# Two tile gates moved to VectorE, and the other gates' matmuls moved between two transposes

## The reference

```
scores = scale * q @ k^T, masked to a window (4 heads) or a dilated window (4 heads)
x      = softmax(scores) @ v                      # 2304 rows of 512
logits = normed(x) @ normed(expert_emb)^T / tau   # 8 experts
e, g   = argmax(logits), softmax(logits)[argmax]
x      = g * (relu(x @ w1[e]) @ w2[e])            # per row, its one expert
h      = x @ w_in
out    = (h * cos(h)) @ w_out
```

## Time and profile before

| | |
|---|---|
| time, median of 3 executions | 856.87 us (856.0 to 858.98) |
| time of the profiled execution | 854.68 us |
| its span, first to last instruction | 852.8 us |
| TensorE busy | 823.2 us, 97% of the span |
| VectorE busy | 608.7 us, 71% |
| ScalarE busy | 489.9 us, 57% |
| GpSimd busy | 75.7 us, 9% |
| mean granted TensorE clock | 0.994 of full speed |

### The profile page before, as it was taken

The page is one execution under the profiler, slowest core; times in us unless marked ns, Lnnn a source line. Parts: engine busy times, 40 slices in busy tenths (PEclk is TensorE's granted clock), DMA queues, the critical chain, the costliest instruction groups (busy, mean ns, idle before and its releaser), DMA issues.

```text
span 852.8 us, 15550 instructions
## 1 busy us (share of the span) xinstructions
PE 823.2 (97%) x5046; PEld 753.6 (88%) x5046; DVE 608.7 (71%) x1187; ACT 489.9 (57%) x948; POOL 75.7 (9%) x129
## 2 busy tenths in 40 slices
PE   7999999989999999999999999999999999999994
PEld 5778787879999999999989999989999998999993
DVE  7888887876555555555577777798777788777762
ACT  4567767644455454444466666676666676666652
POOL 3112112240100000000000000011000003000002
PEclk9999999999999999999999999999999999999998
DMA  7597886255535434434431211223121214122001
GB/s 148 121 223 180 192 192 197 64 151 170 185 124 162 148 123 125 148 128 144 124 100 52 73 63 62 73 89 111 51 75 50 75 49 149 55 70 67 9 1 74
DMA packets 114913, 93.79 MB, mean 110 GB/s; under 512 B 65816, under 2 KB 94488, under 8 KB 114848
## 3 DMA queue, kind: packets, MB, share of 16 engines
q1 hardware_dynamic: 109920, 78.81, 32.5%
q0 software_dynamic: 4928, 14.16, 5.0%
HBM read 83.51 MB, written 9.44 MB: 109 GB/s over the span
## 4 chain that ended last, share of the span: by engine, by line
PE 84%; DVE 6%; issue 3%; DMA 2%; ACT 2%; POOL 1%; another core or an unknown queue 0%; POOLq 0%; DVEq 0%; ACTq 0%; SPq 0%
PE bank L765 24%; PE bank L763 24%; PE bank L764 24%; PE bank L625 2%; PE bank L604 2%; DMA xtok<-x_rows 2%; PE bank L613 1%; PE bank L588 1%; DVE shifted L1271 1%; DVE row_max L1268 1%; PE bank L706 1%; ACT probs L947 1%; PE bank L805 1%; DMA x_rows<-osb 1%; DVE kT L334 1%
## 5 line engine op out<-in xcount | busy, mean ns | idle before, releaser
L763 PE MATMUL bank<-yh,up_l 128*128 128x384 f32 x384 | 129.4, 337 | 0.5 <-DVE yl L1619 0.5
L765 PE MATMUL bank<-yh,up_h 128*128 128x384 f32 x384 | 129.5, 337 | 0.0
L764 PE MATMUL bank<-yl,up_h 128*128 128x384 f32 x384 | 128.9, 336 | 0.0
L765 PE MATMUL bank<-dn_h,hid 128*128 128x512 f32 x288 | 113.9, 396 | 0.0
L763 PE MATMUL bank<-dn_h,hid 128*128 128x512 f32 x288 | 112.5, 391 | 1.4 <-DVE hid L1597 1.4
L764 PE MATMUL bank<-dn_l,hid 128*128 128x512 f32 x288 | 113.8, 395 | 0.0
L1344 DVE TENSOR_TENSOR dn_l<-dn_raw,dn_h 128x512 fp32r<-128x512 f32 (+1 forms) x79 | 71.8, 909 | 54.5 <-ACT dn_h L998 52.5
L1141 ACT ACTIVATE work<-bank 128x384 f32<-128x384 f32 x96 | 47.2, 492 | 79.7 <-PE bank L765 78.7
L998 ACT ACTIVATE dn_h<-dn_raw 128x512 fp32r<-128x512 f32 (+1 forms) x79 | 63.7, 806 | 41.8 <-PE bank L765 41.8
L1153 ACT ACTIVATE work<-work 128x384 f32<-128x384 f32 x96 | 50.5, 526 | 63.8 <-DVE work L1592 61.8
L763 PE MATMUL bank<-xh,up_l 128*128 128x352 f32 x256 | 83.9, 328 | 2.0 <-DVE XS L1479 1.0
(11 more groups left out here) (212 smaller groups left out, 1692.4 us busy)
## 6 DMA issues: line engine op xcount, KB each, us to landing
up_raw<-in_moe_w_dram SPq DMA_DIRECT2D x32, 512.0 KB, 3.6
dn_raw<-in_moe_w_dram SPq DMA_DIRECT2D x32, 512.0 KB, 3.6
up_raw<-in_moe_w_in_dram SPq DMA_DIRECT2D x24, 512.0 KB, 3.4
dn_raw<-in_moe_w_out_dram SPq DMA_DIRECT2D x24, 512.0 KB, 3.6
qn<-in_q_dram SPq DMA_DIRECT2D x32, 144.0 KB, 2.9
kn<-in_k_dram SPq DMA_DIRECT2D x32, 144.0 KB, 3.3
xtok<-x_rows SPq DMA_DIRECT2D x4, 1152.0 KB, 7.6
x_rows<-osb POOLq DMA_DIRECT2D x8, 288.0 KB, 3.5
```

The lines of the kernel that those rows point to most:

```text
L763: mm(o, w[1], x[0], start=first, stop=False, skip_group_check=True)
L764: mm(o, w[0], x[1], start=False, stop=False, skip_group_check=True)
L765: return mm(o, w[0], x[0], start=False, stop=last, skip_group_check=True)
```

## The change

- The gates of tiles 0 and 2 are multiplied in by VectorE, with a `tensor_scalar`, in place of ScalarE. A semaphore `tile_gated_d` tells TensorE of them. Tile 1 and tiles 3 to 17 stay with ScalarE.
- On VectorE `to_gates(to_gate, rest)` goes ahead of `gates_out(head)`, and `ids_out(rest)` stands between the two new gate instructions. The four table instructions come after all of these.
- On TensorE the 24 matmuls with `to_gate` stand between the transposes of tiles 1 and 2, in place of after tile 2. One of the two `fill(1)` is gone.
- On VectorE `expert_up_lo(0, 1)` stands ahead of the wait for, and the read of, the rest's gates.

```
+    BY_VECTOR = (0, 2)
...
             def transpose_rows(tile, b):
-                pe.wait_ge(tile_gated, tile + 1)
+                if tile in BY_VECTOR:
+                    pe.wait_ge(tile_gated_d, BY_VECTOR.index(tile) + 1)
+                else:
+                    pe.wait_ge(tile_gated, tile + 1 - sum(x < tile for x in BY_VECTOR))
...
-            for tile in range(3):
-                transpose_rows(tile, tile)
-                fill((1, 1, 0)[tile])
+            transpose_rows(0, 0)
+            fill(1)
+            transpose_rows(1, 1)
             pe.wait_ge(to_gate_ready, 2)
             for t in range(RT):
                 last = picked(bank[3], to_gate, t, 3 * (ST - HEAD), t == 0, t == RT - 1)
             last.then_inc(row_gates_done, 1)
+            transpose_rows(2, 2)
...
-            gate_rows(0)
             gate_rows(1)
             first_rows_hi(0)
-            gate_rows(2)
             first_rows_hi(1)
             first_rows_hi(2)
...
+            def gate_rows(tile):
+                dve.wait_ge(tile_in[tile], 16)
+                ts(xrow[:, tile, :], xrow[:, tile, :], gates[:, tile:tile + 1], None, ALU.mult).then_inc(tile_gated_d, 1)
+
+            to_gates(to_gate, rest)
+            dve.wait_ge(row_gates_done, 1)
+            gates_out(head, bank[7])
+            dve.wait_ge(gates_ready, 1)
+            gate_rows(0)
+            dve.wait_ge(row_ids_done, 2)
+            ids_out(rest, bank[5])
+            gate_rows(2)
             first_row = base[:, 0:E * RT:RT]
             link(V.memset(table[:], 0))
...
-            dve.wait_ge(row_gates_done, 1)
-            gates_out(head, bank[7])
-            dve.wait_ge(row_ids_done, 2)
-            ids_out(rest, bank[5])
-            to_gates(to_gate, rest)
-
...
             for tile in range(3):
                 first_rows_lo(tile)
+            expert_up_lo(0, 1)
             dve.wait_ge(row_gates_done, 2)
             gates_out(rest, bank[3])
-            expert_up_lo(0, 1)
```

More of the change, by code:

```diff
@@ L239, in fused_kernel @@
         to_row_ready = sem("to_row_ready")
+        tile_gated_d = sem("tile_gated_d")
         lane_sq_ready = sem("lane_sq_ready")
```

## The result

| | before | changed |
|---|---|---|
| time, median of 20 executions | 857.03 us (855.23 to 860.36) | 859.35 us (857.08 to 862.36) |
| ratio, 95% interval | | 1.0026 (1.0014 to 1.0037) |
| span of the profiled execution | 852.8 us | 858.5 us |

The forecast was 855.5 us with a range of 853.8 to 857.3. The change costs about 2.3 us by the medians where a gain of 1.4 was forecast, and the median lies above the range.

The account below looks back on a forecast made before the run. TensorE, busy 97% of the span, was taken as the bound. Up unit 4 was to start 1.4 us earlier (0.15 start, 0.19 and 0.04 up unit 2 and `hid`, 1.04 unit 4): 856.87 to 855.5 us, range 853.8 to 857.3.

Parts of the forecast that it names:

- The matmuls between tiles 1 and 2: On TensorE, 24 `to_gate` matmuls take 0.77 us ahead of tile 2's transposes, which end at 177.86 instead of 178.11.
- What is queued behind that wait: On VectorE, table instructions and three `xl` end at 179.2; first up unit starts at 179.35 against 179.50, gain 0.15.
- Head of VectorE, tile 0: VectorE's `to_gates(rest)` hides in a wait; tile 0's `tensor_scalar` takes 0.43 us, its transposes start 0.27 us earlier.
- The up split, up units 2 and 4: Early `up_l` on VectorE removes TensorE's waits: 0.19 ahead of up unit 2, 0.04 after, 1.04 ahead of up unit 4.
- (a) to (d): Four cases for when VectorE's read of the rest's gates is released: 180.4, 180.9, 182.33 or 183.0.
- (b): Read of the rest's gates comes a fixed lag of 3.65 us behind the `to_gate` matmuls, at 180.9.
- A: The forecast itself: the wait ahead of up unit 4 goes whole; gain 1.4 us, 855.5; chance 0.42.
- B: Unknown wait ahead of the gates' read stays, takes back part; gain 1.1 or 0.5 us, about 856.1; chance 0.22.
- (d): Read of the rest's gates is released with GpSimd's last issue, 182.49 before; then released at 183.0.
- C: VectorE late with first tiles, by tile 2's landing or a slow `tensor_scalar`; gain 0.7 us, 856.2; chance 0.13.
- D: Gain does not reach the end, as something hidden behind 205 us shows; 856.9 us; chance 0.09.
- E: VectorE's gate of tile 2 held through GpSimd's six gathers; experts start 6.8 us later, 5.5 us slower, 862.4; chance 0.06.

Follow-up runs that it names:

- e1: Changed kernel with the 24 `to_gate` matmuls moved back behind tile 2's transposes; ratio to before 0.9967.
- e2: Changed kernel with one `to_gate` matmul in place of 24; ratio to before 0.9973.
- e5: Changed kernel with the 24 `to_gate` matmuls reading 9 columns in place of 45, on the chip without late signals; no ratio, up unit 4 at sorting time 29.77.
- e4: Kernel before with only `expert_up_lo(0, 1)` moved ahead of the wait for and read of the rest's gates; ratio to before 0.9985.
- m3: Changed kernel with GpSimd's gathers of tiles 3 to 8 held until tile 2's transposes are done, and `fill(7)` ahead of the first up unit; ratio to before 0.9963.
- e7: Changed kernel with the `to_gate` matmuls behind tile 2's transposes, `fill(1)` ahead of these and `fill(5)` ahead of the first up unit; ratio to before 1.0014.
- m2: Changed kernel with tiles 3 to 8 brought by plain loads from SyncE's queue in place of GpSimd's gathers; no ratio, first up unit at sorting time 17.34.
- e3: Changed kernel with GpSimd's gathers of tiles 3 to 8 held until tile 2's transposes are done; ratio to before 0.9967.
- j3: Changed kernel with `to_gate` matmuls of 9 columns in place of 45, on a chip with late signals; no ratio, first up unit at sorting time 22.00.
- m1: Changed kernel with a `fill(1)` after every fourth `to_gate` matmul, on a chip with late signals; no ratio, first up unit at sorting time 21.96.
- j1: Changed kernel, unaltered, run again on another chip; ratio to before 1.0040.
- e6: Changed kernel with a `fill(1)` after every fourth `to_gate` matmul, on the chip without late signals; no ratio, first up unit at sorting time 18.30.
- e8: Kernel before with GpSimd's gathers of tiles 3 to 8 held until the `to_gate` matmuls have signalled; ratio to before 1.0023.

## Why the prediction was wrong

**The step that failed** is in "The matmuls between tiles 1 and 2", which put the 24 `to_gate` matmuls ahead of tile 2's transposes at no cost but their 0.77 us. It let ScalarE have tile 2 at the end of its transposes, so that, as "What is queued behind that wait" has it, "its last `xh` would end at 178.45". I had seen the lateness of 3.6 us and carried it as unknown, but pinned it to the gates' read. It belongs to the next signals of TensorE behind the group, whichever they are, and the edit moved the one signal that everything waits for behind the group. In sorting time the last `xh` was to end at 16.2 and ended at 19.8. The row that would have told was at hand in the kernel before, at 183.85 in ScalarE's list: the signal of up unit 0 was late as well, by 2.2 us, so it could not be a matter of the gates. A second term was put at nothing: the half clock behind the break, named as a sign of being wrong but with no price in the sum.

**The size, from the profile.** Late start of the first up unit 3.32, and 1.43 for the half clock (unit 0 takes 3.42 us in place of 1.99). Against this the stretch from up unit 1 to up unit 4 is 2.0 us shorter (10.44 in place of 12.45), for which the forecast had 1.27. 3.32 + 1.43 - 2.0 = 2.75, the whole difference at up unit 4. The three are pieces of one stretch in one pair of profiles, so they must add up; they say where the time went, and the medians of 20 say how much there was, 2.3 us. Of the 2.0 the forecast missed 0.7 because it counted each break as idle time behind the modelled end of the matmul before. By starts, the step from tile 4's transposes to up unit 4 is 1.64 us before (192.30 to 193.94) and 0.36 after (198.75 to 199.11), so that break cost 1.28 and not 1.04; the ones ahead of up unit 2 and down unit 0 were undercounted likewise.

**Head of VectorE, tile 0.** Right within a few hundredths. `to_gate` directly behind the head's part, the gates read at 176.90. The `tensor_scalar` takes 0.49 us, above my 0.43 and just above my upper figure of 0.48. TensorE's transposes of tile 0 start at sorting time 12.97 in place of 13.25: 0.28 earlier, forecast 0.27.

**What is queued behind tile 2.** Right in kind: the second gate stood idle for 1.00 us until the tile landed. In sorting time it started at 14.2, where I had 13.95. With the signals on time the first up unit starts at 17.38 to 17.42 (e1, e2, e5) and not at my 17.1: a loss of 0.15 in place of a gain of 0.15. So this part is a small loss even at its best.

**The up split, up units 2 and 4.** Neither waits in the changed kernel, but partly by luck: TensorE came 3.3 us late and slow itself. In e4, the step alone, the wait ahead of up unit 4 stayed. The release time T of the gates' read, by the semaphore update, is 182.42, or 180.0 on the clock of before, 2.9 us behind the matmuls: none of (a) to (d), though (b) is the nearest in kind. The gain was a share of what the lateness costs. m3, which takes the lateness away, reaches up unit 4 at 29.89, 1.8 us ahead of before. On the chip where nothing was late e7 was 0.1% slower than before, not faster.

**Rivals.** A had the largest chance and fell. B was the nearest in kind, since it kept the late signal, but it had it take back a part of the gain and never asked which other signals stand behind the group. (d) in B, the match with GpSimd's last issue, was a trace of the cause: GpSimd is part of it, though the signals do not wait for the last issue (in the changed kernel ScalarE went on at 183.95 and GpSimd issued until 185.34). C held in a small part, the later landing above, but not with a slow `tensor_scalar`: both gates took 0.49. D did not come up: what was won or lost by up unit 4 is there at the end within 0.6 us. E named the right sign and place, a first up unit starting after 180.8, for a mechanism that was not there and at more than twice the size: 6.8 us late and 5.5 slower, where 3.3 and 2.3 were measured. The clock was named among what would make the prediction wrong, behind a longer break, and so it was.

**The Trainium skill.** "TensorE: Matmul & The Clock Gate", Part 3, has the signal of a group's last matmul arrive about 0.13 us after it. The trace agrees in m2 (ScalarE reads 0.09 us behind it) and disagrees in the changed kernel (3.88 us). I gave it a sentence and used it for nothing; a rule that the row at 182.36 contradicts by a factor of nearly 30 deserved a rival of its own.

**What stays open.** Shown is that it takes the group of short matmuls and gathers issued by GpSimd at the same time (e2, e3, m2), that neither the columns (j3) nor the density as varied (m1) decide it, and that on one chip it did not happen at all. How many matmuls it takes between 1 and 24 was not tried. How the two come to hold up a signal of TensorE is not shown. The half clock is not settled either: it came behind breaks of 1.39 (e1), 1.98 (m2), 1.99 (e3) and 5.0 to 6.6 us (changed, j1, j3, m1), and not behind breaks of 2.00 (e2), 1.99 (e5) and 1.39 (e6), so the length of the break alone does not decide it. It never came with dummies in the break, where m3 with m2 beside it on one chip tells the most. Its price was not measured apart, but it is no accident of one execution: in batch 3 the granted clock of whole executions was 0.989 to 0.994, mean 0.991, in the 12 of the changed kernel and 0.993 to 0.996, mean 0.995, in the 23 of the kernel before.

## What to carry to other kernels

When a wait in the profile has no releaser, find all signals of the same engine around it before you move anything: if two consumers of one engine are late together, suspect the signals of that engine, and expect whatever you put next in its list to be hit. Where you see this, keep long groups of tiny matmuls behind the signals that the critical chain waits for, or keep GpSimd from issuing gathers beside them. And put a control into each batch: an edit that "cures" a fault on a chip that doesn't have it looks the same as a cure.

## What the runs showed of the hardware

- The signal of a group of 24 short matmuls and the first ones behind it were late while GpSimd was issuing gathers: that of the `to_row` group by 1.5 to 2.2 us, that of the `to_gate` group by 2.6 to 5.1, tile 2's behind it by 3.6 to 5.2, up unit 0's, where it ended while that of `to_gate` hung, by 2.2 to 2.8 (semaphore updates). Without the group or without the gathers they were on time (under 0.1 us). The engine's own matmuls went on in the meantime: in the kernel before, unit 0 took its usual 1.99 us, starts 0.16 us apart, while the signal of `to_gate` hung.
- The fault was there in three batches and absent in one, each on another chip. In the one without it the kernel before took 853.21 us, in the others 856.56 to 857.19; how much of this is the fault's is not shown.
- A `tensor_scalar` within the on-chip memory took 1.97 us in place of 0.22 in e8. It began inside an issue of GpSimd that ended at 190.91 and was itself over at 192.29, just behind GpSimd's memset (192.20). "SBUF — State Buffer" of the Trainium skill, section "Who interferes with whom", says that such an instruction and GpSimd block each other for a whole instruction. This row agrees in kind. The second gate of the change does not: it began 0.73 us into an issue (178.14 to 179.08) and took 0.49 like the first, beside which GpSimd was idle.
- The issue in that row took 1.92 in place of 0.95 for another reason: without the delay it would have been over at 189.94, ahead of the `tensor_scalar`. It had begun while VectorE made the low part of a weight pair (188.87 to 190.10). Issues that began inside such an instruction were longer the more was left of it: 1.92 with 1.10 left (e8), 1.49 with 0.67 left (the kernel before, at 222.27), 0.95 with less than 0.1 left. An issue already under way when it began kept its 0.95 (the changed kernel, 184.39).
